# The order of work at the change of head pairs in a banded attention, on three engines

## The reference

```
scores = q @ k^T / 8;  kept where key < n_sink or 0 <= query - key < window, else -1e9
a = exp(scores - max);  a = a / (sum(a) + 1e-9);  x = a @ v      # 1536 tokens x 512
x = relu(x @ w_in) ** 2 @ w_out                                  # 512 -> 2048 -> 512
h = x @ w_in2;  s = h * softmax(h);  ln = (s - mean) / sqrt(var + 1e-6) * g
out = ln @ w_out2                                                # 512 -> 1024 -> 512
```

## Time and profile before

| | |
|---|---|
| median of 3 runs | 498.95 us (497.9 to 500.12) |
| the profiled execution | 499.36 us, span 497.6 us |
| busy in the span | TensorE 481.1 us (97%), VectorE 287.4 (58%), ScalarE 248.0 (50%), POOL 106.7 (21%) |
| granted TensorE clock | 1.00 throughout |
| attention | from the first scores (6.3 us) to the last sums (93.6 us) |

### The profile page before, as it was taken

One profiled execution on the slowest core, in us unless ns is written; L12 is line 12 of the kernel. 1 busy time (PEld: TensorE's weight loads), 2 busy tenths in 40 slices (PEclk: granted clock), 3 DMA queues, 4 the chain that ended last, 5 costly groups with the idle time before them and its releaser, 6 DMA issues.

```text
span 497.6 us, 7811 instructions
## 1 busy us (share of the span) xinstructions
PE 481.1 (97%) x2742; PEld 387.4 (78%) x2742; DVE 287.4 (58%) x678; ACT 248.0 (50%) x539; POOL 106.7 (21%) x129
## 2 busy tenths in 40 slices
PE   6889897999999999999999999999999999999997
PEld 3656575787888888888888888888888888888885
DVE  5788776368677454334435433444497666666651
ACT  3978878433443453344345334434356555545441
POOL 1876666049998000000000000000000000000000
PEclk9999999999999999999999999999999999999999
DMA  6768821170000000000000000000000000000001
GB/s 199 290 238 308 316 98 36 44 297 0 0 0 0 0 1 1 0 0 0 0 1 0 0 1 0 0 0 1 0 1 22 22 21 21 21 21 21 21 28 57
DMA packets 10138, 25.97 MB, mean 52 GB/s; under 512 B 3200, under 2 KB 5248, under 8 KB 8832
## 3 DMA queue, kind: packets, MB, share of 16 engines
q1 hardware_dynamic: 10112, 25.64, 14.1%
HBM read 22.48 MB, written 3.15 MB: 52 GB/s over the span
## 4 chain that ended last, share of the span: by engine, by line
PE 86%; ACT 6%; DVE 3%; DMA 3%; SPq 1%; POOL 1%; issue 1%; DVEq 0%
PE ps L1023 26%; PE ps L1038 26%; PE ps L1073 13%; PE ps L1052 13%; ACT probs L480 3%; PE ps L1059 2%; DMA k_sb<-in_k_t 2%; PE ps L951 2%; PE ps L906 1%; PE ps L915 1%; PE ps L961 1%; ACT pt_sb L488 1%; SPq L320 1%; POOL probs L402 1%; ACT x_hi L494 1%
## 5 line engine op out<-in xcount | busy, mean ns | idle before, releaser
L790 DVE CAST act_hi<-act_sq 128x512 fp32r<-128x512 f32 x48 | 26.0, 542 | 126.1 <-ACT act_sq L538 123.3
L533 ACT ACTIVATE ps<-ps 128x512 f32<-128x512 f32 x48 | 27.9, 582 | 141.4 <-PE ps L1023 141.4
L1023 PE MATMUL ps<-x_hi,w_in_hi 128*128 128x512 f32 x192 | 75.1, 391 | 0.0
L1038 PE MATMUL ps<-act_hi,w_out_hi 128*128 128x512 f32 x192 | 74.8, 390 | 0.1
L1023 PE MATMUL ps<-x_hi,w_in_lo 128*128 128x512 f32 x192 | 74.8, 389 | 0.0
L1023 PE MATMUL ps<-x_lo,w_in_hi 128*128 128x512 f32 x192 | 74.7, 389 | 0.0
L1038 PE MATMUL ps<-act_hi,w_out_lo 128*128 128x512 f32 x192 | 74.7, 389 | 0.0
L1038 PE MATMUL ps<-act_lo,w_out_hi 128*128 128x512 f32 x192 | 74.7, 389 | 0.0
L402 POOL TENSOR_TENSOR probs<-probs,row_inv 128x512 f32<-128x512 f32 (+1 forms) x48 | 45.7, 973 | 30.8 <-DVE row_inv L691 30.8
L480 ACT ACTIVATE probs<-probs,neg_max 128x272 f32<-128x272 f32 (+2 forms) x96 | 46.7, 497 | 7.1 <-DVE neg_max L678 7.0
L1023 PEld LDWEIGHTS ps<-x_hi,w_in_hi 128*128 128x128 f32 x192 | 36.0, 188 | 8.5 <-issue 1.2
(11 more groups left out here) (97 smaller groups left out, 829.3 us busy)
## 6 DMA issues: line engine op xcount, KB each, us to landing
w_in_raw<-in_w_in SPq DMA_DIRECT2D x4, 1024.0 KB, 4.8
w_out_raw<-in_w_out SPq DMA_DIRECT2D x4, 1024.0 KB, 8.2
k_sb<-in_k_t SPq DMA_DIRECT2D x8, 408.0 KB, 5.1
q_sb<-in_q_t SPq DMA_DIRECT2D x8, 384.0 KB, 4.2
v_sb<-in_v SPq DMA_DIRECT2D x16, 192.0 KB, 3.9
out<-out_sb SPq DMA_DIRECT2D x12, 256.0 KB, 2.0
w_in_raw<-in_w_in SPq DMA_DIRECT2D x1, 2048.0 KB, 9.4
w_out_raw<-in_w_out SPq DMA_DIRECT2D x1, 2048.0 KB, 13.8
```

Source lines behind the costliest of these rows:

```text
L533: nc.scalar.activation(ps[:, H_BANK + u, :], ps[:, H_BANK + u, :], ACT.Relu).then_inc(relu_done, 1)
L790: dve.tensor_copy(act_hi[:, u, :], act_sq[:, u, :]).then_inc(act_hi_done, 1)
L1023: last = mm(ps[:, H_BANK + u, :], w[:, u, c, :], x[:, c, t * TILE1:(t + 1) * TILE1], start=(c == 0 and m == 0), stop=(c == DC - 1 and m == 2))
L1038: last = mm(ps[:, Y_BANK + c, :], w[:, u, c * P:(c + 1) * P], a[:, u, :], start=(first and m == 0), stop=(final and m == 2), skip_group_ch ...
```

## The change

At m = 0 of each pair but the first, TensorE does the old pair's products 4 and 5 and the sinks ahead of the new pair's transposes, where they stood behind. ScalarE does the group 0 exponentials of the next pair first, then x_hi, then the copy of the transposes; before, it was x_hi, copy, exponentials. At p = 0 it does the exponentials ahead of the copy. VectorE does the first half of x_lo ahead of its copy and the second half behind it; both stood behind. At m = 1 and m = 2 nothing changes, and no instruction is added or taken away.

```diff
@@ ScalarE, banded_attention
                     for m in range(NG):
-                        if m == 0 and p > 0:
-                            x_high(p - 1)
-                        copy_turned(p, m)
+                        if m > 0:
+                            copy_turned(p, m)
                         if p < LAST:
                             exps(p + 1, m)
+                        if m == 0:
+                            if p > 0:
+                                x_high(p - 1)
+                            copy_turned(p, m)
@@ VectorE
-            def x_low(p):
-
-                for half in range(2):
-                    dve.wait_ge(x_hi_done, 2 * p + half + 1)
-                    dve.tensor_tensor(x_rows(p, x_lo, half), ps[:, X_BANK + half, 0:HALF], x_rows(p, x_hi, half),
-                                      ALU.subtract).then_inc(x_lo_done, 1)
+            def x_low(p, half):
+
+                dve.wait_ge(x_hi_done, 2 * p + half + 1)
+                dve.tensor_tensor(x_rows(p, x_lo, half), ps[:, X_BANK + half, 0:HALF], x_rows(p, x_hi, half),
+                                  ALU.subtract).then_inc(x_lo_done, 1)
@@ VectorE, banded_attention
+                        if m == 0 and p > 0:
+                            x_low(p - 1, 0)
                         copy_turned(p, m)
                         if m == 0 and p > 0:
-                            x_low(p - 1)
+                            x_low(p - 1, 1)
                     if p == 0:
                         w_in_first()
                 chunk(0, 0, 0, 2)
-                x_low(LAST)
+                for half in range(2):
+                    x_low(LAST, half)
@@ TensorE, banded_attention
                     for m in range(NG):
-                        turn_units(p, m)
                         if m == 0 and p > 0:
                             weigh_key(p - 1, 4)
                             weigh_key(p - 1, 5)
                             weigh_sinks(p - 1)
+                        turn_units(p, m)
```

## The result

The changed kernel takes 501.5 us (median of 4 runs, 500.81 to 501.77), the kernel before 498.74 (median of 4). The forecast was "even" at 499.3 with a range of 496.9 to 501.6. The measured time lies 0.1 inside its upper end, and the likeliest case was wrong.

The account below looks back on a forecast made before the run. Bound: a chain of waits across engines in the attention, 9.37 us per pair. New: 5 x 9.45 + 0.3 + 8.55 = 56.10 against 57.70, -1.60; with +1.88 at the first change, +0.28; given as 499.3 us, range 496.9 to 501.6.

Parts of the forecast that it names:

- even: Likeliest case for the whole kernel: new time per pair as long as the old, 499.3 us (497.3 to 501.2), chance 0.76.
- The first change: First change of pairs: exponentials wait for VectorE's late mask, so the second transposes start at 29.56, a loss of 1.88 us.
- The ring: Chain of waits across engines, once per pair in the attention, x_hi to next x_hi: 9.37 us before, 9.45 after.
- VectorE's copy cost 0.32 per pair: Copy behind half of x_lo: second transposes start 1.74 after x_hi, where ScalarE's copy would allow 1.42.
- TensorE's own route to the third transposes: TensorE's work from x_hi to each pair's third transposes: 4.51 us, against 4.53 by VectorE's route.
- The releaser of the second transposes: Sign in each pair: VectorE, not ScalarE, releases the second transposes; they start near 1.74 after x_hi.
- The last change: Last change of pairs, without group 0 exponentials or scores: sums done at 8.5, x_hi at 8.55 us.
- The waits for k_sb: Scores waiting for the k_sb load: today's waits of 0.99 and 0.95 go, except about 0.3 us.
- The clock: Granted clock taken as unchanged at the early TensorE gap of about 2 us; rival of a fall: +8, 507 us, chance 0.02.
- Slower, VectorE's queue: Rival: VectorE's queue sets each pair's third transposes, 0.4 more in five pairs plus 0.3 in loads, 501.6 us, chance 0.11.

Follow-up runs that it names:

- the gap filled: The changed kernel with the last piece of scores ahead of the long TensorE gap (pair 2, piece 2) computed three times over into the same place: 499.14 us, ratio 1.0006.

## Why the prediction came out as it did

- **The first change** was right: second transposes at 29.55, forecast 29.56. ScalarE's exponentials wait there for masks that stand behind w_in_lo, and x_hi and the copy wait behind them. Keeping the old order there gave 3.9 us back, the clock's part among them.
- **The ring** was right in size, 9.45 against 9.44. The single-part runs support its working: with the exponentials out of the way it falls to 8.80, with VectorE's copy first to 8.92. One term was mis-sized. I let VectorE's copy cost 0.32 per pair and gave TensorE's own route to the third transposes the same length as VectorE's; without the split these transposes came 4.06 behind x_hi (47.91 to 51.97) in place of 4.53, and the ring fell by 0.52.
- **The releaser of the second transposes** was right too, though the idle time in their row names ScalarE. In the changed kernel ScalarE's copy had ended at 50.38, and VectorE's ended at 50.71, just ahead of them (50.82):

```profile
49.80 0.58 ACT L488 ACTIVATE pt_sb<-ps 128x512 f32<-128x512 f32 x1
50.03 0.68 DVE L700 COPY pt_sb<-ps 128x512 f32<-128x512 f32 x1
...
52.83 0.66 DVE L700 COPY pt_sb<-ps 128x512 f32<-128x512 f32 x1
```

- **The last change** was right: 8.60 against 8.55.
- **The waits for k_sb**: forecast 0.3 on the ring, measured 0 in the changed kernel, where the slow stretch came first, and 0.53 before the scores with the gap filled.
- **The clock** is the step that failed: "so the sum takes the clock as unchanged". The mechanism stood among the rivals with a chance of 0.02 and a price of 8. It happened in the profiled execution, and all four runs have a mean clock below 1, 0.986 to 0.997. It cost 2.38 in the first x_hi distance and, with the wait for k_sb that it covered, 1.8 in the profiled executions and 2.4 in the medians. I had drawn on one stretch of one execution, 5 to 10 us at clock 1.00, and on the sum of its idle time, 2.41. That sum is made of two gaps with the first scores between them, of which the later, behind them, is 1.08. In that same stretch the changed kernel's profile has the same 14 matmuls, a gap of 2.32 behind the first scores, and a clock of 0.78. The price was too high because I doubled a whole pair: the lower level lasted until 35 us and covered 4.9 us of matmuls, from 29.55 to 34.47, which take 2.77 at the full clock.
- **Slower, VectorE's queue**: its route does stand in front of the third transposes (the copy ends at 53.49, they start at 53.59, 4.53 behind x_hi), but at the length that I had reckoned and not longer. The ring kept 9.44 in the changed kernel.

So "even" was right for the kernel without the fall of the clock, measured at 499.14, and the fall made it slower. (The 499.3 itself is a little rounded up: 499.36 + 0.28 - 0.41 is 499.2.) That 501.5 still lies inside the range is luck: the upper end of 501.6 came from VectorE's rival, which did not happen, and the rival that did was priced at 507.

## What to carry to other kernels

When an order by hand is changed, walk the first and the last turn of the loop as well as the middle: the gain per turn was small here, and the loss sat in the first turn, where other work was in front. Where the new order opens a gap on TensorE (here one of 2.09 us, with one of 0.90 shortly before it), forecast both clock levels, with real weight on the lower one, and price it by the matmuls on the critical path until it recovers. Read single gaps for this, not the idle time summed over a window. Change one engine's order at a time, and then in pairs: of the three parts here one was worth 2.3 to 2.7 us, and the other two gave it back, 0.52 per pair of it only when they stood together.

## What the runs showed of the hardware that I had not expected

The granted clock behind a gap varies from run to run of one kernel: with VectorE's order of before (a gap of 1.71 us in the profile) the mean clock stayed at 1.000 in 5 of 12 runs. The length of that gap alone does not tell. A gap of 0.90 or 0.91 and some scores stand ahead of it. With the gap filled, the scores take 1.65 and the second gap is 1.17; the clock stayed at 1.00. With ScalarE's old order alone, they take 0.73 and the second gap is only 0.65; the clock fell. What decides between the two is not shown.

A fall of the clock need not cost anything. In 43 runs of the kernel before whose clock is on record, 11 had a mean clock of 0.992 or 0.993 and took 497.7 to 499.6 us, like the 23 at 1.000 (497.6 to 499.8). The run with the old order in the first change has a fall in its profile, 0.50 between 10 and 15 us. ScalarE is busy for 4.93 of these 5 us there, and also in the kernel before at 1.00, and the transposes that follow start at 15.68 and 15.77.

Matmuls can also take twice as long while the granted clock reads 1.00: the eight scores of 2.13 us at 16.17, and the twelve first scores, 2.56 in seven of the ten profiles and 1.38 in three. Just those three have the fall in the clock behind these scores. What slows the matmuls stays open. So does the scatter with the old order in the first change: three runs at a mean clock of 1.000 took 498.7 to 498.8 us, the eight below 497.2 to 498.2.
